# Loading, turning and scheduling of the second half-batch in a fused attention, channel-mix and gated-convolution kernel

## What is computed

```python
# 1. attention: 8 heads of 64; heads 0-3 local, heads 4-7 strided
mask_local   = (rel >= 0) & (rel < 32)
mask_strided = (rel >= 0) & (pos_k % 32 == pos_q % 32)
attn = softmax(where(mask, q @ k.T / 8, -1e9)) @ v        # -> x [4, 576, 512]
# 2. channel mix
xk = mu_k * x + (1 - mu_k) * x_prev                       # x_prev: x one position back
xr = mu_r * x + (1 - mu_r) * x_prev
v2 = maximum(xk @ w_k, 0) ** 2 @ w_v                      # w_k [512, 1024], w_v [1024, 512]
x  = sigmoid(xr @ w_r) * v2                               # w_r [512, 512]
# 3. gated convolution over 3 positions
h  = maximum(x @ w_in, 0)
out = (h * sigmoid(conv3(h, conv_w))) @ w_out
```

## Time and profile before

| | before |
|---|---|
| three runs, median (lowest to highest) | 554.48 us (551.88 to 555.55) |
| the profiled execution, own time | 550.11 us |
| its span on the core | 548.3 us |
| granted TensorE clock, mean | 0.993 |
| busy: PE, PE weight loads | 97%, 89% |
| busy: DVE, ACT, POOL | 59%, 52%, 24% |
| moved by DMA | 38.65 MB, mean 70 GB/s |

### The profile page before, as it was taken

One profiled execution on the slowest core, in us unless ns is written; L12 is line 12 of the kernel. 1 busy time (PEld: TensorE's weight loads), 2 busy tenths in 40 slices (PEclk: granted clock), 3 DMA queues, 4 the chain that ended last, 5 costly groups with the idle time before them and its releaser, 6 DMA issues.

```text
span 548.3 us, 15024 instructions
## 1 busy us (share of the span) xinstructions
PE 529.1 (97%) x6114; PEld 486.0 (89%) x6114; DVE 324.3 (59%) x798; ACT 284.0 (52%) x774; POOL 133.7 (24%) x157
## 2 busy tenths in 40 slices
PE   8858999999999999999999999999999999999997
PEld 4546899999999999999999999996998799889976
DVE  5762696756656664756656553996188118806920
ACT  4347829559259187096394450482275127516720
POOL 8036994204004023022023286700000000000000
PEclk9979999999999999999999999999999999999999
DMA  9758423223234143143102405201300130010011
GB/s 213 124 135 216 73 78 64 59 69 65 46 77 73 29 91 65 23 103 75 45 3 101 185 21 176 88 1 39 124 1 1 57 124 0 0 70 7 0 38 57
DMA packets 99442, 38.65 MB, mean 70 GB/s; under 512 B 92596, under 2 KB 92616, under 8 KB 99380
## 3 DMA queue, kind: packets, MB, share of 16 engines
q1 hardware_dynamic: 94484, 29.55, 22.9%
q0 software_dynamic: 2496, 7.66, 4.2%
q10 hardware_dynamic: 2400, 0.59, 0.6%
HBM read 28.33 MB, written 9.44 MB: 69 GB/s over the span
## 4 chain that ended last, share of the span: by engine, by line
PE 80%; SPq 6%; DVE 5%; ACT 2%; issue 2%; POOL 2%; DMA 2%; ACTq 0%
PE ps L700 16%; PE ps L690 14%; PE ps L588 9%; PE ps L589 8%; PE ps L590 8%; PE ps L639 6%; PE ps L640 6%; PE ps L641 6%; SPq L285 5%; PE ps L500 2%; PE ps L545 2%; DVE cbuf L1134 2%; PE ps L533 1%; DMA wv_raw<-in_moe_w_v_dram 1%; DVE wb_hi L1018 1%
## 5 line engine op out<-in xcount | busy, mean ns | idle before, releaser
L439 POOL TENSOR_TENSOR k_lo<-k,k_hi 128x288 fp32r<-128x288 f32 x64 | 60.0, 944 | 179.1 <-ACT k_hi L753 179.0
L1134 DVE SCALAR_TENSOR_TENSOR cbuf<-hbuf,cols_c,cbuf 128x576 f32<-128x576 f32 x64 | 56.4, 883 | 61.1 <-ACT cbuf L843 59.9
L639 PE MATMUL ps<-k_hi,wb_hi 128*128 128x288 f32 x256 | 75.8, 296 | 0.4 <-POOL wb_lo L431 0.4
L640 PE MATMUL ps<-k_lo,wb_hi 128*128 128x288 f32 x256 | 75.5, 295 | 0.0
L641 PE MATMUL ps<-k_hi,wb_lo 128*128 128x288 f32 x256 | 75.4, 295 | 0.0
L588 PE MATMUL ps<-xk_hi,wa_hi 128*128 128x288 f32 x224 | 67.1, 299 | 0.5 <-issue 0.5
L589 PE MATMUL ps<-xk_lo,wa_hi 128*128 128x288 f32 x224 | 66.1, 295 | 0.0
L590 PE MATMUL ps<-xk_hi,wa_lo 128*128 128x288 f32 x224 | 66.1, 295 | 0.0
L700 PE MATMUL ps<-wb_hi,g_hi 128*128 128x512 f32 x144 | 57.8, 401 | 1.2 <-DVE g_lo L1149 1.0
L700 PE MATMUL ps<-wb_hi,g_lo 128*128 128x512 f32 x144 | 56.9, 395 | 0.0
L700 PE MATMUL ps<-wb_lo,g_hi 128*128 128x512 f32 x144 | 56.6, 393 | 0.0
(11 more groups left out here) (107 smaller groups left out, 1217.2 us busy)
## 6 DMA issues: line engine op xcount, KB each, us to landing
x2d<-x2s SPq DMA_DIRECT2D x8, 576.0 KB, 3.1
x2raw<-x2d SPq DMA_DIRECT2D x4, 1152.0 KB, 5.5
out_dram<-ob SPq DMA_DIRECT2D x16, 256.0 KB, 2.0
raw<-in_q_dram SPq DMA_DIRECT2D x112, 36.0 KB, 2.0
raw<-in_k_dram SPq DMA_DIRECT2D x112, 36.0 KB, 2.0
vl<-in_v_dram SPq DMA_DIRECT2D x32, 72.0 KB, 2.1
wk_raw<-in_moe_w_k_dram SPq DMA_DIRECT2D x4, 512.0 KB, 9.6
wv_raw<-in_moe_w_v_dram POOLq DMA_DIRECT2D x4, 512.0 KB, 8.2
```

Source lines behind the costliest of these rows:

```text
L439: nc.gpsimd.tensor_tensor(k2_lo[:, m], k2[:, m % K2RING], k2_hi[:, m].bitcast(F32), ALU.subtract).then_inc(k2_done, 1)
L639: nc.tensor.matmul(dst, wb_hi[:, f, cols], k2_hi[:, f, :], start=(f == 0), stop=False)
L640: nc.tensor.matmul(dst, wb_hi[:, f, cols], k2_lo[:, f, :], start=False, stop=False)
L1134: nc.vector.scalar_tensor_tensor(out=c, in0=h[:, o:o + S], scalar=conv[:, o, m:m + 1], in1=c, op0=ALU.mult, op1=ALU.add).then_inc(conv_ste ...
```

## The change

Half 1's q and k are loaded as half 0's are: `load_rows` gets a half as an argument, SP issues 12 row DMAs in place of 32 `raw` ones (each group waits until half 0's rows in the same buffer are turned), `turn_rows(1, ...)` on PE in slots 1 and 3 of half 0, `lay_q(1, ...)` on ACT in the same slots, `lay_k(1, ...)` on DVE in slots 1 and 4. The four DVE transposes of half 1 are gone. Half 1's steps go by a table of its own, `SECOND`. The turned rows use the banks of scores and values (4 to 7), hence waits for `maxed` and `o_copied`.

w_v, then w_r are issued by SP behind these rows; half 1's v (4 local, 12 strided DMAs) by POOL behind half 0's. The high parts of w_v move to slots 5, 7, 8, 9, the low parts to behind `low_k2` 4, 5, 7 and 7. The waits for low parts of w_v and w_k are split by contraction step.

In front, the strided block of half 0 is normalised ahead of `copy_out(0, 1)` and `mix_k`, its values on PE stand ahead of the first w_k products, values of block 1 follow block 0 directly, and ACT copies out both pairs of the strided result. Some buffers are laid out in another order, and semaphores get names by half.

```diff
     PLAN = ((1, 2, 4, 8), (4, 5, 9, 12))
+    SECOND = ((2, 3, 5, 7), (5, 6, 9, 11))
+    TURN = (1, 3)
     MIX_LOCAL, MIX_STRIDED = 10, 14
...
-        BT = (((0, 1), (2, 6)), ((7, 0), (1, 2)))
+        BT = ((((0, 1), (2, 6)), ((7, 0), (1, 2))), (((4, 5), (6, 7)), ((6, 7), (4, 5))))
...
-            return [i for i, at in enumerate(PLAN) if at[step] == slot]
+        def of_slot(h, step, slot):
+            return [i for i, at in enumerate(SECOND if h == 1 else PLAN) if at[step] == slot]
...
             h0 = HG if strided else 0
+            if c:
+
+                wait(eng, rows_turned, 2 * PAIRS * (strided + 1))
             for i in range(RUNS):
-                src = (q, k)[T][0, h0:h0 + HG, ROWS * i:ROWS * i + ROWS].rearrange("h p d -> p h d")
-                eng.dma_start(rows[:, strided, T, i], src).then_inc(rows_loaded[strided][T], 16)
+                n0 = HALF * c + ROWS * i
+                src = (q, k)[T][0, h0:h0 + HG, n0:n0 + ROWS].rearrange("h p d -> p h d")
+                eng.dma_start(rows[:, strided, T, i], src).then_inc(rows_loaded[c][strided][T], 16)
...
 
-            load_rows(sp, 0, False)
-            load_rows(sp, 0, True)
+            load_rows(sp, 0, 0, False)
+            load_rows(sp, 0, 0, True)
             load_v_local(sp, 0, 0)
+
             for i in range(WK_IN):
                 src, raw_w, _, _ = weights1[i]
                 sp.dma_start(raw_w, src).then_inc(w1_loaded[i], 16)
-            load_raw(sp, 0, 1, False, range(PAIRS))
-            load_raw(sp, 0, 1, True, range(PAIRS))
-            load_v_local(sp, 0, 1)
-            load_v_strided(sp, 0, 1)
+            for strided in (False, True):
+                for T in range(2):
+                    load_rows(sp, 1, T, strided)
+            for i in [*range(WR_IN, WV_IN), *range(WK_IN, WR_IN)]:
+                src, raw_w, _, _ = weights1[i]
+                sp.dma_start(raw_w, src).then_inc(w1_loaded[i], 16)
...
             load_v_strided(pool, 0, 0)
-
-            pool.wait_ge(raw_loaded[1], 16 * RAW_DMAS)
-            for i in range(WK_IN, WV_IN):
-                src, raw_w, _, _ = weights1[i]
-                pool.dma_start(raw_w, src).then_inc(w1_loaded[i], 16)
+            load_v_local(pool, 0, 1)
+            load_v_strided(pool, 0, 1)
...
+            after = {4: (0,), 5: (1,), 7: (2, 3)}
             for m in range(FT):
                 low_k2(0, m)
-                if m % 2 and m // 2 < WV_IN - WR_IN:
-                    low_w1(WR_IN + m // 2)
+                for i in after.get(m, ()):
+                    low_w1(WR_IN + i)
...
-                if h:
+                if h > 1:
                     wait(pe, turned, 4 * h + (2 if kind == LOC else 4))
                 else:
-                    wait(pe, q_laid, PAIRS * (1 if kind == LOC else 2))
-                    wait(pe, k_laid, PAIRS * (1 if kind == LOC else 2))
+                    wait(pe, q_laid, PAIRS * (2 * h + (1 if kind == LOC else 2)))
...
-                if n == block_at(1):
-                    wait(pe, first_copied, 1)
...
+            def turn_rows(c, strided):
+                if c and not strided:
+
+                    pe.wait_ge(maxed, tiles_at(1))
+                    pe.wait_ge(o_copied, block_at(1))
                 for T in range(2):
-                    pe.wait_ge(rows_loaded[strided][T], 16 * RUNS)
+                    pe.wait_ge(rows_loaded[c][strided][T], 16 * RUNS)
+                    if c and strided:
+
+                        if T:
+                            pe.wait_ge(maxed, tiles_at(1, 1))
+                        else:
+                            pe.wait_ge(k_laid, 3 * PAIRS)
                     for pair in range(PAIRS):
-                        if strided and (T or pair):
+                        if not c and strided and (T or pair):
 
...
+                    if low is not None:
+                        pe.wait_ge(w_lo_done, low + t + 1)
                     nc.tensor.matmul(dst, w_hi(t), x_hi(t), start=(t == 0), stop=False)
                     nc.tensor.matmul(dst, w_hi(t), x_lo(t), start=False, stop=False)
                     mm = nc.tensor.matmul(dst, w_lo(t), x_hi(t), start=False, stop=(t == KT - 1))
...
-                    if h == 1 and s == 0:
-                        pe.wait_ge(w_lo_done, WV_IN - WR_IN + WK_IN)
                     cols = slice(P * s, P * s + P)
                     product(bank,
                             lambda t: wa_hi[:, t, cols], lambda t: wa_lo[:, t, cols],
                             lambda t: xk_hi[:, t, :], lambda t: xk_lo[:, t, :],
-                            xk_done if s == 0 else None, KT * h).then_inc(tile_done, 1)
+                            xk_done if s == 0 else None, KT * h,
+                            WV_IN - WR_IN if h == 1 and s == 0 else None).then_inc(tile_done, 1)
...
-                    if h == 0 and n == 0 and part == 0:
-                        pe.wait_ge(w_lo_done, WV_IN - WR_IN)
                     if part == 0:
...
                             wait(pe, k2_done, FT * h + f + 1)
+                            if h == 0:
+                                wait(pe, w_lo_done, f // per + 1)
                         dst = ps[:, n % 4, 0:HALF]
...
             values(0, 0)
-            keep_warm(WARM_SLOT)
             values(0, 1)
-            keep_warm(WARM_SLOT)
+            keep_warm(2 * WARM_SLOT)
+            values(0, 2)
             for m in range(EARLY_M):
                 plain_w_k(m, (0,))
-            values(0, 2)
             for m in range(EARLY_M):
                 plain_w_k(m, range(1, EARLY_T))
 
             for h in range(NH):
                 for slot in range(SLOTS):
+                    if h == 0 and slot in TURN:
+                        turn_rows(1, slot == TURN[1])
                     if h < NH - 1:
...
             act.wait_ge(o_done, block_at(1))
-            src, dst = strided_out(0, PAIRS + 1, ps[:, BO + 1])
-            nc.scalar.copy(dst, src).then_inc(first_copied, 1)
+            for pair in range(PAIRS):
+                src, dst = strided_out(0, PAIRS + pair, ps[:, BO + pair])
+                nc.scalar.copy(dst, src).then_inc(first_copied, 1)
...
                 for slot in range(SLOTS):
+                    if h == 0 and slot in TURN:
+                        lay_q(1, slot == TURN[1])
...
-                        high_w1(WR_IN + slot // 2 - 1)
+                    if h == 0 and slot in (5, 7, 8, 9):
+                        high_w1(WR_IN + (5, 7, 8, 9).index(slot))
                     if h == 0 and slot in (11, 12, 13, 14):
                         high_w1(slot - 11)
...
-                if h == 0 and kind == STR:
-                    src, dst = strided_out(0, PAIRS, ps[:, BO])
-                elif kind == LOC:
+                if kind == LOC:
...
-                if t == PAIRS:
+                if h == 0 and t >= PAIRS:
+                    wait(dve, first_copied, t - PAIRS + 1)
+                elif t == PAIRS:
                     wait(dve, o_copied, block_at(h + 1))
-                if h == 0 and t == PAIRS + 1:
-                    wait(dve, first_copied, 1)
...
+                        k0 = 2 * HALF * pair + HALF * c
+                        dst = kT_s[:, k0:k0 + HALF].rearrange("p (r j) -> p j r", j=JH)
                         src = src.rearrange("p (j r) -> p j r", r=STRIDE)
                     else:
...
             copy_out(0, 0)
+            normalize(0, 2)
             copy_out(0, 1)
             dve.wait_ge(const_turned, P // CR)
             mix_k(0, 0)
-            normalize(0, 2)
             mix_k(0, 1)
-            copy_out(0, 2)
             mix_k(0, 2)
             mix_k(0, 3)
-            turn(1, 1, 0)
-            turn(1, 1, 1)
+
+            dve.sem_inc(o_copied, 1)
 
             for h in range(NH):
                 ahead = h < NH - 1
                 for slot in range(SLOTS):
+                    if h == 0 and slot == TURN[0]:
+                        lay_k(1, False)
+                    if h == 0 and slot == TURN[1] + 1:
+                        lay_k(1, True)
                     if ahead:
...
                         gate_v(h, (slot - 14) // 2)
-                    if h == 0 and slot == 2:
-                        turn(1, 1, 2)
-                        turn(1, 1, 3)
```

More of the change, by code:

```diff
@@ L172, in attention_channel_mix_gated_conv @@
         ident_set = sem("ident_set")
-        rows_loaded = [[sem(f"rows_loaded_{n}_{x}") for x in "qk"] for n in ("local", "strided")]
+        rows_loaded = [[[sem(f"rows_loaded{c}_{n}_{x}") for x in "qk"] for n in ("local", "strided")] for c in range(2)]
         rows_turned, q_laid, k_laid = sem("rows_turned"), sem("q_laid"), sem("k_laid")
@@ L737, in attention @@
             def attention(h, slot):
-                for i in of_slot(1, slot):
+                for i in of_slot(h, 1, slot):
                     exps(h, i)
```

83 lines of the change are left out of this document (40 added, 43 removed).

## The result

| | median us | lowest to highest | profiled execution | its span |
|---|---|---|---|---|
| before, beside it | 553.89 (20 runs) | 551.14 to 557.71 | 550.1 | 548.3 |
| changed | 551.09 (20 runs) | 547.36 to 553.24 | 551.22 | 549.0 |

The ratio is 0.9948, with a 95% interval of 0.9929 to 0.9966: 2.9 us (1.9 to 3.9) less, which is within 1%. The forecast was 6.7 us less, 547.8. 551.09 still lies inside the range of 543.0 to 552.0, but the gain is 2.9 us in place of 6.7, and most of it does not come from the place that was forecast, so the forecast was wrong.

The account below looks back on a forecast made before the run. TensorE, busy 97%, was taken as the bound, with POOL arriving together at half 1's first tile. POOL's end 5.45 us earlier plus 1.2 of cover gave 6.65: 554.5 - 6.7 = 547.8 us, range 543.0 to 552.0.

Parts of the forecast that it names:

- The prologue: First steps, ahead of half 1's turning: half 0's strided values start at about 20.6 and end at 22.1 us.
- TensorE's path: TensorE from 22.1 us: products, two turnings of 1.3 us each, scores, values, w_v; free at 68.4, 9.0 us earlier.
- Does the data come in time?: Half 1's local rows land by 23.7 or 26.3 us, wanted at 27.1; strided wanted at 31.5: no wait, or 1.1.
- ScalarE and POOL: ScalarE's w_v part 1 at 48.15, then POOL without pause to 72.3, gating half 1's first tile: 6.65 us gained.
- POOL's issues: POOL's 16 extra issues cost 0.59 us each, 9.4 in all, to 22.3; hidden, as its first split is wanted at 30.
- Rival 4: Slower: half 1's v loads keep POOL from its splits; 561.7 us at 2.6 us an issue; chance 0.05.
- rival 3: Clock falls around half 1's turning, losing again the 2.1 us of clock counted as won: 549.9 us; chance 0.07.
- The rule weighed there: Transposes don't count as busy for the clock, so the stretch behind each turning call could run low: 549.9 us.

Follow-up runs that it names:

- v_on_sp_held_warm: Changed kernel, half 1's rows held until half 0's last values are issued, four warm matmuls moved back, half 1's v by SyncE behind w_r: 545.48 us, ratio 0.9872.
- v_late: Changed kernel, but POOL issues half 1's v only once half 1's local rows are turned: 552.89 us, ratio 0.9999 to the kernel before.
- old_prologue_timed: Changed kernel with the old order of its first steps alone, timed: 547.93 us, ratio 0.9893 to the kernel before.

## Why the prediction was wrong, point by point

**The prologue** is the step that failed. I costed the strided values at 1.4 us from 20.6 and had them over at 22.1; they were over at 27.5. What failed is the term at nothing: no time for TensorE to get its instructions. The 5.4 us are 3.74 of hole, 0.7 of low clock in the 47 behind it, and 1.3 of the warm matmuls that ran at the low clock in this execution (3.18 for what takes 1.90), less 0.3 by which the first values were early; in the next execution the warm ones were fast and the hole 4.08. I had checked every wait in the program and none of the block that the instructions come in. The row was there to be seen: the DMA view of the kernel before has the instruction packets, and its timeline the same pause at 142.44.

**TensorE's path.** The 20 half products behind the hole, taken at full clock (5.0 us), took 7.18; that is the other 2.2 us of the delay. The two calls of turning took 1.16 and 1.28 (forecast 1.3), the strided scores 1.43 (1.4). From the start of turning to the end of the strided scores are 9.8 us (34.54 to 44.36); the forecast's terms give 10.1 (20 half products 5.0, turning 2.6, scores 2.5).

**Does the data come in time?** Yes, at 34.5 and 38.8 by default, and in v_on_sp_held_warm with 0.5 us of waiting at 26.6 for rows issued only from 21.8 on. But asking only whether the data is in time missed what the traffic does to others: it had room to spare (in v_on_sp_held_warm rows went out from 21.8 on, and turning began 8 us earlier than in the changed kernel, where they went out from 7.7 on), and used it to fill the engines when the instructions were due.

**ScalarE and POOL.** Right in its lengths: 24.0 us from part 1 on (24.15), POOL the gate and TensorE waiting for it 0.7 us inside the tile and 1.9 for `wb_lo`, where I had 0.3. Parts 2 and 3 took 6.65 and not 5.6, w_k's pieces 12.48 and not 13.4. Only the start moved, from 48.15 to 55.19.

**POOL's issues**: 4 in 2.45 us and 12 in 6.99, 0.6 each beside VectorE. Rival 4 fell; the case that the Trainium skill warns of in SBUF — State Buffer, section SBUF: two separate sides, did not arise here (its 0.62 and 3.1 us are for a whole DMA, not, as the prediction has it, for an issue). Rival 4's mechanism itself is real, as v_late shows when the issues are put where POOL is wanted.

**The clock and the turning** (rival 3). The clock fell, but in and behind the hole, and in the first execution also ahead of it, from 18.1 to 21.5 us, among the warm matmuls; neither is near the turning. From 34 to 43 us, both calls of turning in it, it is 1.00, and in v_on_sp_held_warm 1.00 from 20 to 30 with turning at 26.58. The rule weighed there, of the Trainium skill, TensorE: Matmul & The Clock Gate, Part 4: PE-mode transpose, cost nothing in this kernel.

**Where the 2.9 us come from.** Not from the edit's own place: the scores of half 2 start at 79.88 and 79.08 against 79.65 and 79.81, 0.25 us earlier in the mean. The pause at 141.5 (0.94 and 1.38 us, 1.22 and 1.10 in two variants of the kernel before) is gone, because the blocks end elsewhere: 1.2 us. Behind it the clock fell to 0.91 for 20 us in two of the four executions, 1.8 us each time; but one variant of the changed kernel (old_prologue_timed) shows that dip too, without a pause. 0.25 + 1.2 + up to 0.9 is 1.5 to 2.4 of 2.9. Two numbers of the timed runs bear on the rest. What lies around the span is 2.3 us in the changed kernel (2.2 to 2.5 in 20 runs) and 1.8 before (45 runs), so the gain inside the span is 3.4, and 0.5 of it is lost outside; the variants with the v of half 1 on SyncE have 1.8 to 1.9. And the mean granted clock is 0.9897 against 0.9884, which by an estimate (share of the span not granted) is 0.8 us. The rest is open; that the dip belongs to the pause is argued, not shown, and which part of the gain is due to where the blocks end is not measured by a run.

**Left open**: why TensorE goes on only about 3 us behind the packet (2.4 to 2.7 at 141 us, with the DMA engines nearly idle, share 0.12 and 0.18 from 138 to 144), and what asks for a packet. In all 17 executions it comes after TensorE has entered the block before, as if that entry asked for it; no run tests this.

## What to carry to other kernels

Ahead of moving loads forward, look for rows with the releaser "issue" in the middle of one line's matmuls, and at the instruction packets in the DMA view: 88 of the short matmuls take 1.4 us, so a block of some 126 lasts 2.0, less than the 2.4 to 3.5 us between a packet and going on, and the packet needs the DMA engines that early loads have filled. Hold loads until they are wanted (a wait in the queue that issues them cost nothing here and gave 4 us), keep longer work between stretches of short matmuls, and don't put the issues on an engine that is the gate later. And don't read a small difference between two kernels as the edit's own worth before the pauses elsewhere are compared: adding 20 tiny matmuls moved one pause and turned one of under 0.6 us into 3.1 us.

## What the runs showed of the hardware that was not expected

- A pause of TensorE without any wait, 0.25 to 4.08 us, at a fixed count of instructions, every 256 of them; 20 matmuls more move it by exactly 20. The Trainium skill, in the section named above, calls the cost of crossing a block mostly hidden; here the measurement decides, and it is up to 4.08 us.
- A 16 KB instruction packet is recorded 1.7 and 2.1 us behind TensorE's entry into the block before (at 17.8 and 18.0) when nothing of half 1 is queued, and 5.2 to 8.3 us behind it (at 20.8 to 23.8) behind the small packets of two queues, 1.18 MB of rows and 0.59 MB of v.
- The granted clock falls in some executions where TensorE is never idle (0.96 from 280 to 320 us in five of seventeen, 1.6 us each). Over 45 executions of the kernel before the mean granted clock runs from 0.982 to 0.994 and the time from 556 to 550 us, mostly in step (correlation 0.89): much of the spread from run to run is clock.
